# Attention, MLP and expert layer in one kernel: scaled tiles, state updates, diagonals and one weight load of the first group at other places

## What is computed

```python
def _attn_ref(r, k, v, w, u):
    for t in range(S):
        cur = einsum('bhd,bhe->bhde', u[None] * kt, vt)
        y[:, :, t] = einsum('bhd,bhde->bhe', rt, state + cur)
        state = w[None, :, :, None] * state + einsum('bhd,bhe->bhde', kt, vt)

def _moe_ref(x, w_in, w_out):          # 384 -> 2048 -> 384
    h = x @ w_in
    g = np.maximum(0.01 * h, h)
    return g @ w_out
```

## Time and profile before

| | us |
|---|---|
| median of 3 runs | 735.33 |
| lowest and highest of them | 731.72, 738.29 |
| the profiled execution | 734.31 |
| its span, first to last instruction | 732.6 |
| TensorE busy in it | 689.9 |
| mean granted TensorE clock | 0.979 |

### The profile page before, as it was taken

How to read it: one execution, slowest core, us unless ns; L and a number is a source line. 1 busy time by engine, 2 the same in 40 slices (tenths; PEclk the granted TensorE clock), 3 DMA queues, 4 the chain that set the end, 5 groups by cost and what they waited for, 6 DMA issues and landing times.

```text
span 732.6 us, 14146 instructions
## 1 busy us (share of the span) xinstructions
PE 689.9 (94%) x4365; PEld 650.5 (89%) x4366; DVE 405.9 (55%) x839; ACT 307.1 (42%) x665; POOL 105.0 (14%) x120
## 2 busy tenths in 40 slices
PE   7977999999999999999999999999998899998973
PEld 7877999999999999999999999999994788987773
DVE  8654565755665565466466545533557352745741
ACT  4434544333444442444443344433442453646530
POOL 6330000010010001001000100100103152344321
PEclk9998999999999999999999999999998999999997
DMA  8645342312422132242204222006015762383200
GB/s 243 200 137 193 121 132 72 99 40 59 130 65 66 36 108 59 60 130 65 66 22 118 63 60 87 12 13 235 1 62 197 285 227 106 111 293 126 100 19 8
DMA packets 38681, 77.44 MB, mean 106 GB/s; under 512 B 8568, under 2 KB 26902, under 8 KB 38624
## 3 DMA queue, kind: packets, MB, share of 16 engines
q1 hardware_dynamic: 33632, 62.37, 27.4%
q10 hardware_dynamic: 2432, 9.76, 3.6%
q0 software_dynamic: 2560, 4.58, 2.0%
HBM read 61.09 MB, written 12.41 MB: 100 GB/s over the span
## 4 chain that ended last, share of the span: by engine, by line
PE 84%; DVE 4%; ACT 4%; issue 4%; ACTq 1%; DVEq 1%; POOL 1%; DMA 1%; POOLq 0%; SPq 0%
PE bank L687 28%; PE bank L705 26%; PE bank L825 6%; PE bank L779 5%; PE bank L569 4%; PE bank L625 3%; PE bank L620 2%; PE bank L764 2%; PE bank L638 2%; PE bank L806 1%; PE bank L663 1%; ACT w_hi L1038 1%; PE bank L607 1%; DVE h_sb L1202 1%; ACT h_sb L920 1%
## 5 line engine op out<-in xcount | busy, mean ns | idle before, releaser
L1202 DVE TENSOR_TENSOR h_sb<-h_sb,bank 128x384 f32<-128x384 f32 x128 | 70.8, 553 | 173.3 <-ACT h_sb L920 172.9
L920 ACT ACTIVATE h_sb<-bank 128x384 f32<-128x384 f32 x128 | 62.8, 491 | 246.8 <-PE bank L687 242.8
L687 PE MATMUL bank<-x_hi,win_hi 128*128 128x384 f32 x384 | 135.6, 353 | 2.7 <-DVE win_lo L1224 1.6
L705 PE MATMUL bank<-wout_hi,g_hi 128*128 128x394 f32 x384 | 131.7, 343 | 0.0
L705 PE MATMUL bank<-wout_lo,g_hi 128*128 128x394 f32 x384 | 131.2, 342 | 0.0
L705 PE MATMUL bank<-wout_hi,g_lo 128*128 128x394 f32 x384 | 131.2, 342 | 0.0
L687 PE MATMUL bank<-x_hi,win_lo 128*128 128x384 f32 x384 | 130.5, 340 | 0.0
L687 PE MATMUL bank<-x_lo,win_hi 128*128 128x384 f32 x384 | 130.3, 339 | 0.0
L1563 POOL DMA_INDIRECT id_list<-idgate,dst x24 | 24.2, 1007 | 480.2 <-DVE dst L1307 475.3
L1209 DVE TENSOR_TENSOR g_lo<-h_sb,g_hi 128x384 fp32r<-128x384 f32 x128 | 70.9, 554 | 33.4 <-ACT g_hi L927 32.3
L927 ACT ACTIVATE g_hi<-h_sb 128x384 fp32r<-128x384 f32 x128 | 66.7, 521 | 42.9 <-DVE h_sb L1202 40.5
(11 more groups left out here) (187 smaller groups left out, 993.0 us busy)
## 6 DMA issues: line engine op xcount, KB each, us to landing
raw<-in_experts SPq DMA_DIRECT2D x32, 768.0 KB, 6.1
rkt<-in_rk_t SPq DMA_DIRECT2D x46, 192.0 KB, 3.6
rkn<-in_rk_nat SPq DMA_DIRECT2D x21, 384.0 KB, 4.1
v<-in_v_nat SPq DMA_DIRECT2D x24, 192.0 KB, 2.8
z_rows<-z_sb SPq DMA_DIRECT2D x24, 192.0 KB, 2.8
out<-z_sb SPq DMA_DIRECT2D x24, 192.0 KB, 2.8
stage<-in_win ACTq DMA_DIRECT2D x4, 768.0 KB, 4.6
stage<-in_wout_t ACTq DMA_DIRECT2D x4, 768.0 KB, 6.1
```

What stands on the lines that cost most here:

```text
L687: mm = pe.matmul(h_ps[t % 2][:, 0:GT], a[:, kk, cols], b[G % 2][:, kk, :], start=n == 0, stop=n == 3 * KT - 1)
L705: mm = pe.matmul(z_ps[i][:, 0:ZW], a[t % 3][:, tok], b[:, f, :], start=f == 0 and j == 0, stop=f == FT - 1 and j == 2)
L920: act.activation(h_sb[t % 2][:], h_ps[t % 2][:, 0:GT], ACT.Copy, scale=SLOPE).then_inc(s_h_scaled, 1)
L1202: dve.tensor_tensor(h_sb[t % 2][:], h_sb[t % 2][:], h_ps[t % 2][:, 0:GT], ALU.max).then_inc(s_leaky, 1)
```

## The change

Four things, all in the first group.

- `LOADS`: of quarters 1 to 3 the `gate` load now stands ahead of `win`. So quarter 1 of `win` goes to buffer 1, whose last reader was `gate_products(0)`, and quarter 1 of `gate` to buffer 0, whose last reader was `low_in_first(3)`. The issues are at other places too: `win` 1 where load 3 was, `wout` 1 behind `high_g(1)`, `gate` 1 in step 0 behind `set_diag(3)`.
- ScalarE: `high_in(1)` and `set_diag(3)` stand in step 0 behind `scale_h(2)`. The halves of `set_diag(4)` stand one step later each, in steps 3 and 4.
- VectorE ahead of step 0: `scale_r(3)` and `scale_k(3)` before `leaky(0)`, `leaky(1)` before `low_g(0)`, the state updates and `sum_diag(3)` before `low_g(1)`, `low_in_first(3)` last.
- VectorE: `update_state(3)` in step 3 behind `leaky(5)`, where it stood first in step 4.

```diff
-LOADS = [(kind, q) for q in range(4) for kind in ("win", "gate", "wout")]
+LOADS = [("win", 0), ("gate", 0), ("wout", 0)]
+LOADS += [(kind, q) for q in range(1, 4) for kind in ("gate", "win", "wout")]
@@ ScalarE
             high_gates(0)
-            load_stage(3)
+            load_stage(LOADED["win", 1])
             scale_h(1)
             high_g(1)
-            load_stage(4)
-            load_stage(5)
-            set_diag(3, range(H))
+            load_stage(LOADED["wout", 1])
 
             for step in range(STEPS):
                 if step % FT == 0 and step > 0:
                     out_z(step // FT - 1)
-                if step in (1, 5, 9):
+                if step in (5, 9):
                     high_in((step + 3) // 4)
                 if step + 2 < STEPS:
                     scale_h(step + 2)
+                if step == 0:
+                    high_in(1)
+                    set_diag(3, range(H))
+                    load_stage(LOADED["gate", 1])
                 n = BEGUN_AT.get(step - 2)
                 if n is not None:
                     out_y(n)
                 n = BEGUN_AT.get(step + 2)
-                if n is not None and n > CPG:
+                if n is not None and n > CPG + 1:
                     set_diag(n, range(4))
                 n = BEGUN_AT.get(step + 1)
                 if n is not None and n > CPG:
-                    set_diag(n, range(4, H))
+                    set_diag(n, range(4) if n == CPG + 1 else range(4, H))
+                if BEGUN_AT.get(step) == CPG + 1:
+                    set_diag(CPG + 1, range(4, H))
@@ VectorE
             low_in_first(1)
+            scale_r(3)
+            scale_k(3)
             leaky(0)
+            low_in_first(2)
             low_out(0)
-            low_in_first(2)
-            low_in_first(3)
+            leaky(1)
             low_g(0)
             low_gates(0)
-            leaky(1)
-            low_g(1)
             for n in range(CPG):
                 update_state(n)
-            scale_r(3)
-            scale_k(3)
             sum_diag(3)
+            low_g(1)
+            low_in_first(3)
@@ VectorE, in the loop over the steps
                 n = BEGUN_AT.get(step - 3)
-                if n is not None and n < CHUNKS - B:
+                if n is not None and CPG < n < CHUNKS - B:
                     update_state(n)
                 if step in (1, 5, 9):
                     low_in((step + 3) // 4)
                 if step + 2 < STEPS:
                     leaky(step + 2)
+                if BEGUN_AT.get(step - 2) == CPG:
+                    update_state(CPG)
```

## The result

| | before | after |
|---|---|---|
| median, first comparison | 736.77 us (6 runs) | 729.31 us (6 runs) |
| profiled execution | 734.31 us, span 732.6 | 726.07 us, span 724.3 |

The ratio is 0.990 with an interval of [0.986, 0.9939]: 7.5 us by the medians. The same kernel was compared twice more, and gave 0.9919 [0.9879, 0.996] and 0.9859 [0.9816, 0.9901]. So the change makes the kernel about 1% faster, 5 to 10 us by the three pairs of medians. The forecast was 8.7 us and 726.6; the median of 729.31 lies in the range. The first ratio's interval reaches to both sides of the 1% mark.

A forecast was written before the change was run, and what follows sets the result against it. TensorE was taken as the bound, with four first-group waits (8.9 us) and half clock after them. 4.3 + 4.1 + 2.3 - 1.7 - 0.3 = 8.7 us off gave 726.6 us by the median, range 720.7 to 731.5.

The forecast's parts named there:

- where I took 0.3: At gate_products(1): a cost of 0.3 us for the gate quarter's landing, with ends of 0 and 3.1.
- 0.1 us to spare: At scores(4): update_state(3) done 1.6 us behind the end of hidden(5), hidden by project(3)'s 1.7 us.
- Step 4: At hidden(4): win 1 issued near 29.8, landing at 34.4; start 42.1 against 46.39, 4.3 us won, wait 2.1 us.
- The port rival: Before hidden(3): GpSimd's two products push low_in_first(3) past 37, hidden(3) waits 0.5 to 1.0 us; 727.6 us; chance 0.08.
- the distance at `project(4)`: The lead of 8.7 us at project(4), to be found again at 130; otherwise the prediction is wrong.
- Terms 1.6 and 2.3: Half clock avoided: 1.6 us from scores(3) to project(1), 2.3 us from scores(4) to project(4).
- The 1.7: Behind the wait at hidden(4): a clock fall, 3.4 us at half clock, costing 1.7 us; ends nothing or 2.5.
- The 4.3 us forecast up to `hidden(4)`: Gain up to hidden(4): start at 42.1 instead of 46.39.
- Late weights: At hidden(4): win quarter lands after 8.2 us, wait 5.5 us, clock down; 729.8 to 730.6 us; chance 0.17.
- the clock's share at 2.5 us: Behind the late-landing wait at hidden(4): clock down as after the 4.10 us wait, costing 2.5 us.
- Slower: ScalarE's step 0, high_in(1) waiting for its quarter: slower from a landing 13.3 us after issue; 736 at 14 us; chance 0.03.
- Given back: Slack runs out or later groups have a hidden bound: 729.8 us, or 732.3 if the tail takes more; chance 0.10.

The follow-up runs named there:

- split gates: Gate products of quarters 2 and 3 in two halves: in the changed kernel 0.983 and, repeated, 0.9866; in the kernel before 1.0012; ratios to the kernel before.
- both edits: Changed kernel with low_in(1) before low_g(2) on VectorE and the gates of quarters 2 and 3 in halves: ratio 0.9875 to the kernel before, median 726.88 us.
- the old buffers: Changed kernel with win 1 back in buffer 0, issued first in step 0, high_in(1) behind set_diag(3): ratio 1.0013 to the kernel before, median 739.04 us.
- gates cut: Changed kernel with two thirds of the gate matmuls of quarters 2 and 3 left out: 735.49 us, not comparable as the routing differs.

## Why the prediction was right, and where it was not

**The steps of the first group held.** From the first `hidden` to the gate products of quarter 2 the kernel before takes 51.1 and 50.6 us in its two profiles and the changed one 41.8, 41.3 and 41.1: 9 to 10 us won, 8.7 forecast (some 6 of them with half clock taken out, the rest clock). Point by point, with 0.86 added for the earlier start: `scores(3)` at 35.25 (forecast 35.5); `scores(3)` to the end of `project(1)` 4.6 us (4.5); `hidden(4)` at 41.75 (42.1) with a wait of 1.89 (2.1); `scores(4)` to `project(4)` 57.01 - 54.25 = 2.76 (2.75); `project(4)` at 57.9 (58.4). The gate quarter was in time in the three profiles of the changed kernel: no wait where I took 0.3 (with other edits there are 0.18, 0.60 and 0.93). `update_state(3)` had not 0.1 us to spare but 0.21 too little.

**Step 4 named the wrong last link.** I had the wait at `hidden(4)` as ScalarE's: landing, `high_in(1)`, `set_diag(3)`, gate load, `high_g(2)`. The load was issued 2.3 us earlier than I thought (27.50 against 29.8): it goes out as soon as the waits ahead of it in the queue are met, the last of them for `leaky(0)`, which ends at 27.46, while L862 still runs from 26.90 to 28.40 and `high_g(0)` and `high_gates(0)` have yet to run. So the quarter was there before `high_in(1)`. ScalarE ended `set_diag(3)` at 37.1 and then waited 0.87 us for VectorE's `leaky(2)`, late since `off` and `idgate` took 0.96 and 1.01 us instead of 0.15 and 0.18, beside GpSimd's products. The experiment with `low_in(1)` early moved VectorE's order alone and the wait was gone, with TensorE late in that profile. My number came out since the two chains end within 0.9 us of each other.

**The port rival happened and cost little.** The rows:

```profile
33.81 1.21 POOL L1555 TENSOR_TENSOR ruk<-rkn 128x384 f32<-128x384 f32 x1 [1.23 <-DVE diag L1153]
...
35.10 1.20 POOL L1557 TENSOR_TENSOR ruk<-ruk,u_sb 128x384 f32<-128x384 f32 x1
```

`low_in_first(3)` took 1.38 us against 0.55, `off` and `idgate` 0.96 and 1.01. What the Trainium skill says in "SBUF — State Buffer", section "SBUF: two separate sides" of a VectorE operation with two SBUF inputs fits `low_in_first(3)`. The same section names operations in a two-port mode beside them; whether `off` and `idgate`, with one input each, ran in one, the profile doesn't say. `hidden(3)` was held by 0.07 us at most (35.58 behind `scores(3)`, which ends 35.55), so nothing of the 1.0 us I gave it was lost there; it came out in the wait at `hidden(4)`, within the 0.9 us above. In the second profile with split gates, whose order up to there is the changed kernel's, `hidden(3)` did wait 0.46 us for this piece, with both edits 0.25, with the old buffers 0.66. So the rival's 0.5 to 1.0 us is met in some executions.

**The failed statement is that nothing behind step 4 changes.** I wrote that the distance at `project(4)` should be found again at 130, and that the prediction is wrong if it is not. The first ranking matmul, L715 before and L716 after (one row of each line's view, with the first and last start):

```profile
L715 PE MATMUL bank<-cum,const x16: 191/274/421, 137.9 to 552.4; 128*128 128x32 f32 x16
...
L716 PE MATMUL bank<-cum,const x16: 191/274/422, 130.7 to 545.2; 128*128 128x32 f32 x16
```

That is 7.2 us, 2.9 less than at `project(4)`, and 6.3 without the 0.86 of the earlier start. The two new stretches at half clock cost 1.7 us each. The end takes 1.1 more off, 8.3 in the span. From the first `hidden` to this matmul the profiles of before have 10.2 us of half clock each, those of the changed kernel 10.2, 10.7 and 10.1: the change moved the half clock there and removed none. 24 matmuls of 9 columns run in one piece for 2.7 us; the two new stretches follow such a piece. They are there in four of four profiles that have the changed order complete with whole gates, at both quarters, and once, at quarter 2, with the old buffers. They are absent in the four of before (two), of before with the diagonals alone and of after with them put back, and in the five with gates cut or in halves. That splitting takes them away is shown by the profiles, in the changed order four with whole gates and four without; why the order before escaped them with the same piece of gates is not. The distance from `scores(4)` is not the reason, as the diagonals alone show. Four profiles of each order make chance unlikely but don't exclude it; nothing here shows what else it is.

**The clock terms of the sum didn't average out as written.** Terms 1.6 and 2.3 were read from one profile, and in the profile they came. The 1.7 came in the first profile of the changed kernel alone; in its other two the clock is 1.00 behind that wait. Over many executions the median clock rose only from 0.973 to 0.975, which is worth 1.5 us (0.002 x 730), where the sum had 1.6 + 2.3 - 1.7 = 2.2. The waits themselves gave 7.0 us in the profile (0.88 + 2.23 + 3.89) less 0.24, and 5.5 us in span times clock over all runs. 1.5 + 5.5 = 7.0 agrees with the measured 5 to 10. Of the 1.3 us between 5.5 and 6.8, 0.9 is the half clock that began at 60.3, 1.7 us before the 4.10 us wait ended, which this figure counts by half; the rest is not accounted for. And the 1.6 was no cost of its own: from `scores(3)` to `hidden(4)` the order before takes 7.75 us with the half clock and, in the run with split gates, without it, since the wait at `hidden(4)` grows by what the clock saves. The 4.3 us forecast up to `hidden(4)`, 4.6 measured, were won because ScalarE and VectorE came through earlier. So that the median is within 3 us of 726.6 is in part luck: the clock terms were right for one profile and little of them is in the average.

**The rivals.** "Late weights" had the right place and too small a price: with the old buffers the wait was 6.1 us, and I had put the clock's share at 2.5 us where the 0.53 of 46 to 58 is 5.6 us ((1 - 0.53) x 12). With that price the case ends at 0.8 + 6.4 - 5.6 = 1.6 us off, no longer at 4.7. The run itself ended 1.5 us over before. Under "Slower" I called 8.2 us the longest transfer; the tile view of the earlier trace rows has one of 10.5. "Given back" was right in kind: 3.4 us, by the clock in a later stretch, not by a hidden bound. The slower case did not occur.

## What to carry to other kernels

Take a load's place and the order of the engines behind it as one change: with the old buffers put back, and with them the places of the issues and of `high_in(1)`, the rest of the change was worth nothing in time. Changes at different waits can add up instead: the diagonals and the rest moved span times clock by 3.4 and 2.7 us alone and by 5.5 together. Where an instruction waits for a late event, look at what is queued behind it on its engine; two half sets of diagonals moved by one step took a 4 us wait from another engine. Half clock ahead of a wait for another engine may cost nothing, since the wait takes it up. And price a stretch at half clock from several executions, since a stretch that leaves one place in one profile may come back in another, where TensorE is never idle.

## What the hardware showed beside

- TensorE goes to 1.2 GHz for 3.4 us with no idle time at all, 1.2 us behind a dense run of 24 matmuls of 9 columns: busy 4.00 of 4.00 us in 66 to 70, clock 0.57 in 70 to 74. Why the kernel before has the same run without a fall is open.
- 13.7 us at half clock began in a wait of 6.1 us, 10.2 us followed one of 3.2, 3.4 to 6.8 came with those of 4.1, and 3.4 with three of four waits of 2.1 to 2.3; behind the fourth the clock stayed up. Of the waits before `hidden(4)`, it stayed up behind five of 1.0 to 1.7 us and fell for 3.4 us after four of 1.8 to 1.9, each time only behind the gate products that follow; once it fell there after waits of 1.3 and 0.9.
- A load on ScalarE's queue was issued at 27.50, before three activations ahead of it had ended or begun (L862 until 28.40, L928 from 28.30, L869 from 28.71): it is held by the waits ahead of it, not by the work.
- A VectorE copy of 128x24 took 1.01 us instead of 0.18 beside GpSimd, and `low_in_first(3)` 1.37 to 1.40 instead of 0.55 in every profile with the new order.
